# Sign projections in 64x32 tiles of the array, products every second step, and one transfer for each raw tile

## The reference

```python
q_bits = (np.einsum('bhsd,dk->bhsk', q, proj) > 0)      # proj: 64 x 6
k_bits = (np.einsum('bhsd,dk->bhsk', k, proj) > 0)
q_bucket, k_bucket = the six bits as a number
mask = q_bucket[:, :, :, None] == k_bucket[:, :, None, :]
scores = np.where(mask, q @ k.T / 8, -1e9)
attn = exp(scores - max); attn = attn / (sum + 1e-9)
out = attn @ v
```

## Time and profile before

| | |
|---|---|
| median of 3 runs | 775.95 us (775.22 to 778.45) |
| the profiled execution: its own time | 775.0 us |
| its span in the trace | 773.0 us |
| mean granted TensorE clock | 0.921 |
| PE busy | 669.9 us, 87% of the span |
| attention (first score to last normalising) | 20.2 to 281.6 us of the span |

### The profile page before, as it was taken

One profiled execution on the slowest core, in us unless ns is written; L12 is line 12 of the kernel. 1 busy time (PEld: TensorE's weight loads), 2 busy tenths in 40 slices (PEclk: granted clock), 3 DMA queues, 4 the chain that ended last, 5 costly groups with the idle time before them and its releaser, 6 DMA issues. The chain is left out here.

```text
span 773.0 us, 10437 instructions
## 1 busy us (share of the span) xinstructions
PE 669.9 (87%) x3758; PEld 536.1 (69%) x3759; DVE 421.8 (55%) x563; ACT 339.9 (44%) x528; POOL 334.3 (43%) x204
## 2 busy tenths in 40 slices
PE   2899999999999979306799999999766899979998
PEld 1766666666666659306699988998544688768886
DVE  5767868677686421512455455652259985542222
ACT  2666666666666623103255334551145454622200
POOL 3552835638351125361464446650056636633300
PEclk9899999999999985556989999999978999989999
DMA  7603370633706026244746667611162202122311
GB/s 175 165 2 100 113 211 11 202 91 121 211 7 233 1 96 253 87 163 137 247 156 209 212 240 244 237 62 56 58 244 68 68 1 69 55 82 82 109 42 55
DMA packets 51504, 96.10 MB, mean 124 GB/s; under 512 B 17152, under 2 KB 17152, under 8 KB 51456
## 3 DMA queue, kind: packets, MB, share of 16 engines
q1 hardware_dynamic: 49536, 89.16, 35.7%
q0 software_dynamic: 1920, 6.29, 2.3%
HBM read 69.23 MB, written 26.21 MB: 123 GB/s over the span
## 5 line engine op out<-in xcount | busy, mean ns | idle before, releaser
L880 POOL TENSOR_TENSOR w_lo<-stage,w_hi 128x1024 fp32r<-128x1024 f32 x28 | 85.2, 3060 | 91.6 <-ACT w_hi L875 91.6
L242 ACT COPY probs_t<-turned 128x768 f32<-128x768 f32 x96 | 76.7, 799 | 72.1 <-PE turned L417 70.8
L306 DVE TENSOR_REDUCE neg_max<-scores 128x1 f32<-128x768 f32 x96 | 91.6, 955 | 26.0 <-PE scores L408 21.9
L250 ACT ACTIVATE probs<-scores,neg_max 128x768 f32<-128x768 f32 x96 | 87.0, 906 | 23.9 <-DVE neg_max L306 23.9
L429 PE MATMUL pv<-probs_t,v_in 128*64 128x384 f32 x384 | 82.3, 510 | 0.9 <-DVE out_t L313 0.8
L969 PE MATMUL up<-xt_hi,w_hi 128*128 128x256 f32 x256 | 75.4, 295 | 8.1 <-issue 6.1
L417 PE MATMUL turned<-ident,probs 128*128 128x128 f32 x576 | 79.7, 275 | 0.6 <-ACT probs_t L242 0.6
L969 PE MATMUL up<-xt_hi,w_lo 128*128 128x256 f32 x256 | 74.8, 292 | 0.0
L969 PE MATMUL up<-xt_lo,w_hi 128*128 128x256 f32 x256 | 74.8, 292 | 0.0
L417 PEld LDWEIGHTS turned<-ident,probs 128*128 128x128 f32 x576 | 69.2, 142 | 6.3 <-issue 2.9
L1307 PE MATMUL y<-z_hi,wt_hi 128*128 128x512 f32 x144 | 57.9, 402 | 8.9 <-POOL wt_lo L1091 6.0
(11 more groups left out here) (196 smaller groups left out, 1455.0 us busy)
## 6 DMA issues: line engine op xcount, KB each, us to landing
stage<-in_w SPq DMA_DIRECT2D x64, 512.0 KB, 4.6
wt_raw<-in_w_tok SPq DMA_DIRECT2D x12, 768.0 KB, 4.5
x_slots<-zeros SPq DMA_DIRECT2D x7, 1024.0 KB, 6.8
y_slots<-zeros SPq DMA_DIRECT2D x7, 1024.0 KB, 8.7
q_raw<-in_qT SPq DMA_DIRECT2D x32, 192.0 KB, 4.2
k_raw<-in_kT SPq DMA_DIRECT2D x32, 192.0 KB, 4.5
x_in<-x_slots SPq DMA_DIRECT2D x10, 512.0 KB, 5.2
y_slots<-y_out SPq DMA_DIRECT2D x8, 512.0 KB, 2.8
```

The source lines that it names most:

```text
L242: nc.scalar.copy(probs_t[j % 2][:, a, :, t % 3 * P:(t % 3 + 1) * P].rearrange("k (b n) q -> k b n q", b=2), turned[:, :, 0:HALF].rearrange ...
L250: nc.scalar.activation(probs[g % 3][:].rearrange("p (b n) -> p b n", b=2), scores[g % 2][:, :, 0:HALF], ACT.Exp, bias=neg_max[:, pair, a, ...
L306: nc.vector.tensor_reduce(neg_max[:, pair, a, t:t + 1], scores[g % 2][:, :, 0:HALF], AX.XY, ALU.max, negate=True).then_inc(s_max, 1)
L880: name.tensor_tensor(w_lo[w][:, r, :], stage[:, r, :], w_hi[w][:, r, :].bitcast(F32), ALU.subtract).then_inc(done, 1)
```

## The change

1. The block `setup` goes. POOL makes identity and zeros at the start of the attention block, where it also fills `ones`. The unread copy goes.
2. A raw tile is loaded by one transfer whose source is the head's 64 rows with a leading dimension of 2 of stride zero. proj is loaded in the same way. For the first pair SP issues q and ACT issues k.
3. The projections read `q_raw` (rows 0 to 63) and `k_raw` (rows 64 to 127) in f32, without the split. One weight tile of 12 columns serves. Head and half choose the column tile of 32: the four results of a pair stand in rows 0, 32, 64 and 96 of `side`. Steps n = 5 (q) and n = 7 (k) each make all four.
4. `products` are made two at a time in odd steps.
5. DVE reads the signs of head 0 in steps 5 and 7, of head 1 in steps 6 and 8. Before the first score they come in pieces of 384 columns (before: 768), so there are eight in place of four.
6. Waits for the prepared tiles move from the projections to the first two scores of a pair. SP waits for the projections of pair p before it loads pair p + 2.

```diff
-SIGNS_AT = {2: (0, 0, 0), 4: (0, 0, 1), 5: (0, 1, 0), 6: (0, 1, 1), 7: (1, 0, 0), 8: (1, 0, 1), 10: (1, 1, 0), 11: (1, 1, 1)}
+Q_AT, K_AT = 5, 7
...
+    def load_rows(engine, raw, src, pair, a):
+        engine.dma_start(raw[pair % 2][a][:], src[2 * pair + a:2 * pair + a + 1, :, :].to_broadcast([2, D, S])).then_inc(
+            s_qk[pair % 2][a], 16)
...
-        sp.dma_start(proj_raw[0:D, :], proj).then_inc(s_const_ld, 16)
-        sp.dma_start(proj_raw[D:P, :], proj).then_inc(s_const_ld, 16)
+        load_rows(sp, q_raw, qT, 0, 0)
+        sp.dma_start(proj_raw[:], proj.unsqueeze(0).to_broadcast([2, D, NBITS])).then_inc(s_const_ld, 16)
+        load_rows(sp, q_raw, qT, 0, 1)
         def load_qk(pair, a):
-            p = pair % 2
-            for raw, src in ((q_raw[p][a], qT), (k_raw[p][a], kT)):
-                for half in range(2):
-                    sp.dma_start(raw[half * D:half * D + D, :], src[2 * pair + a, :, :]).then_inc(s_qk[p][a], 16)
+            load_rows(sp, q_raw, qT, pair, a)
+            load_rows(sp, k_raw, kT, pair, a)
...
             if pair + 2 < NPAIRS:
+                sp.wait_ge(s_z, 2 * pair + 4)
...
     def _(act):
         for a in range(2):
-            act.wait_ge(s_qk[0][a], 64)
+            load_rows(act, k_raw, kT, 0, a)
+        for a in range(2):
+            act.wait_ge(s_qk[0][a], 32)
...
-        def signs(pair, a, of_k, src, cols, n):
+        def signs(pair, a, of_k, src):
             aug = (q_aug, k_aug)[of_k][pair % 2][a]
-            nc.vector.tensor_scalar(aug[BITS:KAUG, cols], src, thresh[of_k][BITS:KAUG, :], (-1.0, MISMATCH)[of_k],
-                                    ALU.is_gt, ALU.mult).then_inc(s_bits, n)
+            for half in range(2):
+                at = 64 * a + 32 * half
+                nc.vector.tensor_scalar(aug[BITS:KAUG, half * HALF:half * HALF + HALF], src[at:at + 2 * NBITS, 0:HALF],
+                                        thresh[of_k][at:at + 2 * NBITS, :], (-1.0, MISMATCH)[of_k],
+                                        ALU.is_gt, ALU.mult).then_inc(s_bits, 1)
...
-                    if n in SIGNS_AT:
...
+                    if n in (Q_AT, K_AT):
+                        dve.wait_ge(s_z, 2 * pair + 4 + n // K_AT + 1)
+                    if n in (Q_AT, Q_AT + 1, K_AT, K_AT + 1):
+                        signs(pair + 1, (n - Q_AT) % 2, n // K_AT, side)
...
-        def project(pair, a, of_k, half, dst):
-            x = (q_hl, k_lh)[of_k][pair % 2][a]
-            for part in ("hi", "lo"):
-                last = nc.tensor.matmul(dst, w_bits[f"{'qk'[of_k]}_{part}"][:], x[:, half * HALF:half * HALF + HALF],
-                                        start=part == "hi", stop=part == "lo")
+        def project(pair, heads, of_k, dst):
+            rows = slice(of_k * D, of_k * D + D)
+            for a in heads:
+                for half in range(2):
+                    at = 64 * a + 32 * half
+                    last = nc.tensor.matmul(dst[at:at + 2 * NBITS, 0:HALF], w_bits[rows, :],
+                                            (q_raw, k_raw)[of_k][pair % 2][a][rows, half * HALF:half * HALF + HALF],
+                                            start=True, stop=True, tile_position=(of_k * D, at))
             last.then_inc(s_z, 1)
...
             if 0 <= g - T_LAG < STEPS:
                 turn(g - T_LAG)
-            if 0 <= g - PV_LAG < STEPS:
-                products(*divmod(g - PV_LAG, 6))
-            if pair + 1 < NPAIRS and n in SIGNS_AT:
-                a, of_k, half = SIGNS_AT[n]
+            if 0 <= g - PV_LAG < STEPS and g % 2 == 1:
+                for m in (g - PV_LAG - 1, g - PV_LAG):
+                    products(*divmod(m, 6))
+            if pair + 1 < NPAIRS and n in (Q_AT, K_AT):
                 side_free(g)
...
+                for a in range(2):
+                    pe.wait_ge(s_qk[(pair + 1) % 2][a], 32 * ((pair + 1) // 2) + 32)
+                project(pair + 1, range(2), n // K_AT, side)
```

More of the change, by code:

```diff
@@ L36, with attention @@
 TURN_LAG = 15
-SIGNS_AT = {2: (0, 0, 0), 4: (0, 0, 1), 5: (0, 1, 0), 6: (0, 1, 1), 7: (1, 0, 0), 8: (1, 0, 1), 10: (1, 1, 0), 11: (1, 1, 1)}
-def attention(nc, ctx, qT, kT, v, proj, x_all, ident, load_routing, clear):
+Q_AT, K_AT = 5, 7
+def attention(nc, ctx, qT, kT, v, proj, x_all, ident, zeros, load_routing, clear):
     def sb(name, shape, dt=F32):
@@ L164, in _ @@
     def _(pool):
+        nc.gpsimd.memset(ident[:], 0.0).then_inc(s_constp, 1)
+        pool.wait_ge(s_constp, 1)
+        nc.gpsimd.affine_select(out=ident[:], in_=ident[:], compare_op=ALU.not_equal, fill=1.0, base=0,
+                                pattern=[[-1, P]], channel_multiplier=1).then_inc(s_constp, 1)
         nc.gpsimd.memset(ones[:], 1.0).then_inc(s_constp, 1)
+        nc.gpsimd.memset(zeros[:], 0.0).then_inc(s_constp, 1)
         def q_high(pair, a):
@@ L266, in const @@
             ins.then_inc(s_const, 1)
[L268 to L273, removed]
-        dve.wait_ge(s_const, n_const[0])
[L275 to L283, removed]
+        for n in range(4):
+            const(nc.vector.memset(thresh[0][n * 32:n * 32 + 32, :], -TINY))
+            const(nc.vector.memset(thresh[1][n * 32:n * 32 + 32, :], 0.0))
+        dve.wait_ge(s_const, n_const[0])
+        for n in range(4):
+            const(nc.vector.memset(thresh[0][n * 32:n * 32 + NBITS, :], 0.0))
+            const(nc.vector.memset(thresh[1][n * 32:n * 32 + NBITS, :], -TINY))
+        dve.wait_ge(s_const_ld, 16)
+        for rows, first_sign in ((slice(0, D), 1.0), (slice(D, P), -1.0)):
+            for at, sign in ((0, first_sign), (NBITS, -first_sign)):
+                const(nc.vector.tensor_scalar(w_bits[rows, at:at + NBITS], proj_raw[rows, :], sign, None, ALU.mult))
         assert n_const[0] == N_CONSTS
@@ L349, in _ @@
                                         ALU.subtract).then_inc(s_klo, 1)
[L350 to L353, removed]
+            for of_k in range(2):
+                dve.wait_ge(s_z, 2 * a + of_k + 1)
+                signs(0, a, of_k, (side, pv)[of_k])
         for g in range(STEPS + TURN_LAG):
@@ L443, in _ @@
         pe.wait_ge(s_const, N_CONSTS)
-        pe.wait_ge(s_constp, 1)
+        pe.wait_ge(s_constp, 3)
         for a in range(2):
-            pe.wait_ge(s_qlo, a + 1)
-            for of_k, dst in enumerate(((scores[0], scores[1]), (turned, scores[0]))[a]):
-                if of_k == 1:
-                    pe.wait_ge(s_khi, a + 1)
-                    pe.wait_ge(s_klo, a + 1)
-                if (a, of_k) == (1, 1):
-                    pe.wait_ge(s_bits, 2)
-                for half in range(2):
-                    project(0, a, of_k, half, dst[0:KAUG, half, 0:HALF])
+            pe.wait_ge(s_qk[0][a], 32)
+            for of_k in range(2):
+                project(0, (a,), of_k, (side, pv)[of_k])
         for g in range(STEPS + TURN_LAG):
@@ L1371, in _ @@
                 tokens(8 + n // 2)
-def setup(nc, ctx, ident, ident_r, zeros):
-    s_ident = ctx.enter_context(nc.semaphore("i_ident"))
-    block = ctx.enter_context(nc.Block())
-    @block.gpsimd
-    def _(pool):
-        nc.gpsimd.memset(zeros[:], 0.0)
-        nc.gpsimd.memset(ident[:], 0.0).then_inc(s_ident, 1)
-        pool.wait_ge(s_ident, 1)
-        nc.gpsimd.affine_select(out=ident[:], in_=ident[:], compare_op=ALU.not_equal, fill=1.0, base=0,
-                                pattern=[[-1, P]], channel_multiplier=1).then_inc(s_ident, 1)
-    @block.vector
-    def _(dve):
-        dve.wait_ge(s_ident, 2)
-        nc.vector.tensor_copy(ident_r[:], ident[:])
 def build(nc, qT, kT, v, proj, w_gate, w_local, w1, w2, w_theta, w_tok, w_ch, out):
@@ L1411, in build @@
             zeros = routed.enter_context(nc.sbuf_tensor("zeros", [P, DM], F32, side="right"))
-            with ExitStack() as ctx:
-                setup(nc, ctx, ident, ident_r, zeros)
             x_all = routed.enter_context(nc.sbuf_tensor("x_all", [P, T, B * DM], F32, side="right"))
@@ L1432, in build @@
             with ExitStack() as ctx:
-                attention(nc, ctx, qT, kT, v, proj, x_all, ident, load_routing, clear)
+                attention(nc, ctx, qT, kT, v, proj, x_all, ident, zeros, load_routing, clear)
             weights = expert_weights(nc, tokens)
```

40 lines of the change are left out of this document (13 added, 27 removed).

## The result

The changed kernel takes 875.51 us (median of 4, 873.14 to 876.99), the kernel before 775.59 in the same session (774.00 to 778.45): a ratio of 1.128, 95% interval 1.124 to 1.133. It is 100 us slower, where 870 was forecast. The profiled execution has 874.36 us and a span of 872.6.

What follows compares the result with a forecast made beforehand. PE, busy 87% of the span, was taken as the bound. From 775.0 us, -7.6 for start and pairs, +95.5 for two-engine transfers and +6 for clock gave 868.9, so 870 us; range 764 to 905, the forecast's own 850 to 905.

Steps and rivals of the forecast that it cites:

- The transfers: Loads of q and k: outermost count 2 gives two engines, 50 GB/s; attention ends 95.5 us later; chance 0.58.
- PE waiting in n = 5 by some 10 us: Sign that the forecast is right: in each pair PE waits that long for k_raw before the projections.
- The round: Attention, later pairs: PE's steps, v's issue and share, latency and transfer make 41.8 us, replacing a pair's 31.5.
- the clock: PE in the attention: below full clock after idling, 1 us a round, 6 us in all (0 to 15).
- Projections: PE, steps n = 5 and 7: four side by side cost 0.8 us a burst, 1.6 us for each pair.
- Products in twos: PE, odd steps: merging saves 0.35 us, but a wait in even steps makes two steps 4.84 us, not 4.72.
- The start: Set-up and first loads: with all DMA engines, first score at 17.0 instead of 20.2 us, -3.2 us.
- first rival: Loads of q and k: all 16 engines serve the doubled source, 768 us, between 764 and 773; chance 0.30.
- Pairs 1 to 6: Attention without transfer stalls: each pair 31.5 us in place of 32.3, six times 0.8, -5.0 us.
- the end: Last pair of the attention: it has no projections to lose and pays 1.1 us.

Runs made afterwards that it cites:

- old_doubled: The kernel before with one change alone: each raw tile loaded by one transfer whose source repeats the 64 rows as its outermost dimension; 872.7 us.
- rows_62_2: two_copies with each 64-row half of a raw tile loaded as 62 rows and 2 rows in two transfers; 875.2 us, one run.
- two_copies: The changed kernel with every raw tile, and the projections' columns, loaded as two transfers of 64 rows, as in the kernel before; 772.8 us.
- rows_57_7: two_copies with each 64-row half of a raw tile loaded as 57 rows and 7 rows in two transfers; 785.2 us, one run.
- twice_in_hbm: The changed kernel with q and k rows stored twice in HBM, one plain 128-row transfer per raw tile, the projections' columns in two transfers; 770.0 us.
- single_products: two_copies with the merging of products undone, one key tile in every step; expected 5 us less and 1 us less at the end; 767.3 us.
- even_slots: two_copies with the bursts of projections at steps 6 and 8 and the output's transpositions one step later, in even steps; 762.7 us.
- paired: two_copies with two steps reordered: both scores, one transposition, products of two key tiles, the other transposition; ACT and DVE in matching order; 769.4 us.

## Why the prediction was right

**The transfers: right, in mechanism and size.** 50 GB/s over two engines, as forecast; old_doubled and rows_62_2 show that it alone suffices, two_copies that nothing else of the change stalls for a transfer. Step by step: DVE took up head 1 of pair 0 at 34.97 (34.7 forecast), first score 41.13 (43.1), first bursts of pairs 1 and 2 at 66.72 and 104.89 (landings at 66.0 and 102.5), pair 7 at 320.77 (311.5). two_copies, without stalls, asks for pair 7 at 220.76 us (216). Only the sign "PE waiting in n = 5 by some 10 us" was too high: it waits 3.4 us there in the mean, after 3.6 us in the other stall. SP's issues show the pace, 7.63 us for a tile of 393 KB:

```profile
2.13 19.65 SPq L121 DMA_DIRECT2D q_raw<-in_qT  x2
21.82 9.52 SPq L121 DMA_DIRECT2D k_raw<-in_kT  x1
31.39 7.63 SPq L121 DMA_DIRECT2D q_raw<-in_qT  x1
39.06 7.63 SPq L121 DMA_DIRECT2D k_raw<-in_kT  x1
```

**The round: 1.4 us too short**, the mis-sized term. The round was 5.6 us from PE's release to the end of n = 7, and 36.2 from the issue of v to the landing. Over the five rounds from 104.89 to 320.77 the first part takes 8.4, 7.0, 8.2, 8.4 and 6.8 us, 7.75 in the mean, the second 35.4: 43.2 in place of 41.8. The 5.6 were summed at full clock, and without stalls they are right (5.6 us in two_copies from 95.48). In the changed kernel PE works at the lower level for most of this part. Three of the five rounds begin so, as here; in the other two the first burst still takes 0.83 us and the fall comes within 2 us (7.0 and 6.8 us):

```profile
234.75 1.47 PE L391 MATMUL side<-q_raw,w_bits 64*12 64x384 f32 x8 [2.50 <-DMA k_raw<-in_kT]
236.15 1.01 PE L419 MATMUL scores<-k_aug,q_aug 76*128 76x384 f32 x2
...
237.59 1.48 PE L428 MATMUL turned<-ident,probs 128*128 128x128 f32 x6
```

At full clock the burst takes 0.83 us and the others 0.62 and 0.82. In the round before this one, the granted clock in the window from 190 to 195 us is 0.54, so mostly the lower of its two levels, 1.2 of 2.4 GHz; PE had idled 4.7 us in the first stall and 2.7 in the second. So the clock, put into the forecast as 6 us at the end of the sum, sits inside the round, where it holds back the next transfer. The second part is 0.8 us shorter than its 36.2, which hides some of it. Pair 7 lands 9.3 us later than forecast, 2.4 of them there at pair 2 and 7 from the five rounds; from its landing to the end of the attention are 62.5 us, 2.2 more than forecast. Less the 6 already counted, that makes the 5.5 by which 870 falls short.

**Projections: right.** Four run side by side: eight records in 0.83 us, and a step with a burst is 0.76 us longer (3.79, not 3.03); 0.8 was forecast. rows_57_7, two_copies and twice_in_hbm all have pairs of 31.32 us; 31.5 were forecast.

**Products in twos: right on the steps, too large for a pair.** Even steps take 1.80 us and two steps 4.83 (4.84 forecast), in place of 4.70 in single_products. That the merge is given back, and a little more, holds: single_products is 5.6 us faster. But six times 0.12 us would be 0.7 in a pair, and the pairs differ by 0.19 (31.32 and 31.13), as the single order has a wait of 0.5 us for DVE's output copy that the merged one lacks. That 5.6 comes close to an expected 5 + 1 is in part luck. The wait itself is 0.28 us and not 0.46: in the even step scores and transposes behind each other take 1.52 us, not the 1.35 that I added up, while the distance was read from a row and was right.

**The start: wrong, but the sum didn't rest on it.** The first rival's 768 us is measured in two_copies as 772.8, and 4 us of the difference are the start. Forecast was a first score at 17.0; it is at 21.12 there (20.2 in single_products, even_slots and paired, which start alike, so 0.9 us is chance), because ACT has q only at 7.55 (6.8 there) and not at 5.4, and because DVE waits for the projections' columns, which the change put behind the first q tile:

```profile
8.83 0.51 DVE L289 TENSOR_SCALAR w_bits<-proj_raw 64x6 f32<-64x6 f32 x4 [6.94 <-DMA proj_raw<-in_proj]
```

PE, idle for 9.3 us before its first score, also starts slowly: 1.01 us for two scores, 0.62 before in the earlier trace rows. That is their length at the lower level; the granted clock reads 1.00 here, but its records in this trace begin only at 31.26 us, and at 31.35 the matmuls have their full-clock lengths. The first pair loses 1.1 us where it was to save 0.5. Pairs 1 to 6 give -6.1 us (-5.0 forecast), the end +1.06 (+1.1). twice_in_hbm has the landing of the forecast, ACT's first work at 5.07, with DVE's wait for the columns to 6.33 and the first score at 18.62. What it tells: the 5.4 needs 128 rows in one transfer over all engines; transfers of 64 rows move 202 GB/s at a share of 1.00, 128 rows 287 at 0.96. The prediction also reads the clock of the earlier trace rows one slice off: it is below full in the second slice, not the third (0.82 from 19.30 to 38.65 us); nothing in the sum hangs on the place.

**Not foreseen:** the first of the two stalls, by way of POOL and DVE. It adds little if anything to the round, which ends with head 1's landing, but it takes half of PE's idle time and brings a fall of the clock of its own (0.68 from 175 to 180 us). It would have shown if the prediction had followed head 0's landing by itself, and not only that of both heads.

## What to carry to other kernels

Before two transfers are made one, look at the outermost count of the new access pattern: here a repeat put in front turned 16 engines into 2, at the same bytes and half the issues, while 128 rows in one transfer were faster than two of 64. A price per tile says little by itself: measure it against the time that hides it, where 3 engines cost 12 us and 2 cost 103. Work that is taken off the busiest engine is worth what the next wait leaves of it; find that wait (here 1.80 us past a single buffer) and put something into it, or order the work around it, and then look at what stands in front of the maximum on the in-order engines behind.

## What the runs showed of the hardware

- How fast a DMA engine is depends on the transfers. Two moved 50 GB/s at a share of 0.13, into 128 partitions and (rows_62_2) into 64, 25 GB/s each; a row of 3 KB took 124 ns in the median, and just as long with three (rows_57_7). All 16 moved 287 GB/s at a share of 0.96 with 128-row transfers (121 ns a row), but 202 at 1.00 with 64-row transfers (215 ns a row), 12.6 GB/s for each busy engine. So 64 partitions alone don't slow an engine, nor do 16 engines alone; both together do, and the busy share then hides a limit that isn't the engines' own. Which one was not tried.
- The engine that issues a transfer is held while many bytes are ahead of it: SP's issue of a tile takes 0.5 us at first in a round and 7.63 us behind other tiles at the start, which is about the time of one tile at 50 GB/s, and in a round at 167 us two clears behind such tiles 12.28 and 3.74 us. It looks like a queue that is full. Work behind an issue on that engine is delayed by it. A small load suffers too: the projections' columns, issued at 1.56 us, reached DVE only at 25.34 us.
- Clock: in each round the granted clock falls twice. In windows of 5 us within or behind a stall it is 0.50 (235 to 240 us), 0.54 (190), 0.68 (175) and 0.71 (150), and the steps from the second stall's end to n = 7 take 7.75 us in place of 5.6. A stall of PE costs more than its own length.
